# Attention and FFN kernel: the first pair's row maxima taken in two parts, and the query sums moved to the ends of odd halves

## The reference, cut to what matters

```python
def _attn_ref(q, k, v):              # q, k, v: 4 x 8 x 1152 x 64
    q_pool = q.reshape(B, H, S // 2, 2, D).mean(axis=3)
    scores = scale * np.matmul(q_pool, k.transpose(0, 1, 3, 2))
    scores = scores - np.max(scores, axis=-1, keepdims=True)
    attn = np.exp(scores)
    attn = attn / (np.sum(attn, axis=-1, keepdims=True) + 1e-09)
    return np.matmul(attn, v)
...
x = attn_out.transpose(0, 2, 1, 3).reshape(B * S, H * D)     # 2304 x 512
h = x @ w_in                                                  # 512 x 2048
g = np.where(h > 0.0, h, np.exp(np.minimum(h, 0.0)) - 1.0)
x = g @ w_out                                                 # 2048 x 512
logits = x @ phi                                              # 32 slots
```

## Time and profile before

| | |
|---|---|
| median of 3 executions | 971.53 us (969.62 to 973.15) |
| the profiled execution, its own time | 970.04 us |
| its span, from the first to the last instruction | 968.3 us |
| start to the first score (L528) | 25.49 us |
| attention | to about 475 us |
| PE, DVE, ACT, POOL busy, share of the span | 95%, 54%, 41%, 37% |

### The profile page before, as it was taken

The page is one execution under the profiler, slowest core; times in us unless marked ns, Lnnn a source line. Parts: engine busy times, 40 slices in busy tenths (PEclk is TensorE's granted clock), DMA queues, the critical chain, the costliest instruction groups (busy, mean ns, idle before and its releaser), DMA issues.

```text
span 968.3 us, 16639 instructions
## 1 busy us (share of the span) xinstructions
PE 918.9 (95%) x6450; PEld 704.1 (73%) x6450; DVE 520.5 (54%) x918; ACT 395.6 (41%) x733; POOL 362.3 (37%) x263
## 2 busy tenths in 40 slices
PE   3999999999999999999999999999999999999794
PEld 2556665656555666565799999999999999999332
DVE  6767666767676667665464443443433433434333
ACT  2655555555555555547442322322322322322102
POOL 1788878787887787888200000000000000000000
PEclk9999999999999999999999999999999999999998
DMA  6022022221211222302330000200000000457895
GB/s 231 25 75 71 30 73 74 75 72 52 75 59 41 74 75 74 91 1 70 105 111 1 1 1 1 88 1 1 1 1 1 1 1 1 144 218 257 310 376 196
DMA packets 36127, 76.32 MB, mean 79 GB/s; under 512 B 2897, under 2 KB 11217, under 8 KB 36049
## 3 DMA queue, kind: packets, MB, share of 16 engines
q1 hardware_dynamic: 36048, 75.26, 22.3%
HBM read 70.53 MB, written 4.72 MB: 78 GB/s over the span
## 4 chain that ended last, share of the span: by engine, by line
PE 49%; POOL 2%; DVE 1%; ACT 0%; DMA 0%; issue 0%; POOLq 0%; ACTq 0%; DVEq 0%
PE psum L611 7%; PE psum L593 7%; PE psum L595 7%; PE psum L612 7%; PE psum L613 7%; PE psum L594 7%; POOL acc L1258 2%; PE psum L688 2%; PE psum L723 1%; PE psum L644 1%; PE psum L650 1%; PE psum L626 0%; PE psum L544 0%; DMA out<-ob 0%; PE psum L631 0%
## 5 line engine op out<-in xcount | busy, mean ns | idle before, releaser
L1258 POOL TENSOR_TENSOR acc<-acc,pt 128x576 f32<-128x576 f32 x220 | 312.6, 1421 | 64.1 <-ACT pt L810 39.0
L810 ACT ACTIVATE pt<-psum 128x576 f32<-128x576 f32 x288 | 182.8, 651 | 135.3 <-PE psum L531 135.2
L530 PE MATMUL psum<-qs,kraw 64*128 64x288 f32 x576 | 182.8, 403 | 0.0
L531 PE MATMUL psum<-qs,kraw 64*128 64x288 f32 x576 | 182.7, 403 | 0.0
L984 DVE TENSOR_REDUCE mx<-psum 128x1 f32<-128x512 f32 x256 | 162.2, 677 | 18.0 <-PE psum L496 16.7
L544 PE MATMUL psum<-pt,vs 128*64 128x288 f32 x1152 | 153.6, 412 | 0.0
L1150 DVE TENSOR_SCALAR gf<-gf 128x384 f32<-128x384 f32 x96 | 34.6, 360 | 195.7 <-ACT gf L926 195.7
L611 PE MATMUL psum<-gh,W 128*128 128x384 f32 x384 | 133.4, 347 | 0.0
L926 ACT ACTIVATE gf<-psum 128x384 f32<-128x384 f32 x96 | 47.2, 492 | 200.8 <-PE psum L595 200.2
L612 PE MATMUL psum<-gl,W 128*128 128x384 f32 x384 | 128.5, 335 | 0.0
L595 PE MATMUL psum<-xh,W 128*128 128x384 f32 x384 | 128.5, 335 | 0.0
(11 more groups left out here) (128 smaller groups left out, 1324.3 us busy)
## 6 DMA issues: line engine op xcount, KB each, us to landing
ring<-in_w SPq DMA_DIRECT2D x32, 1024.0 KB, 7.4
qraw<-in_qT SPq DMA_DIRECT2D x16, 576.0 KB, 4.9
kraw<-in_kT SPq DMA_DIRECT2D x16, 576.0 KB, 3.7
vs<-in_v SPq DMA_DIRECT2D x16, 576.0 KB, 3.8
out<-ob SPq DMA_DIRECT2D x9, 512.0 KB, 6.2
wst<-in_w_in SPq DMA_DIRECT2D x16, 256.0 KB, 2.8
wst<-in_w_out SPq DMA_DIRECT2D x16, 256.0 KB, 3.1
sel<-in_selection SPq DMA_DIRECT2D x1, 96.0 KB, 6.8
```

Source lines behind the costliest of these rows:

```text
L530: mm(lo, kraw[0:64, p % NB, keys], qs[0:64, p % NB, q], start=False, stop=True).then_inc(s_Ta, 1)
L531: mm(hi, kraw[64:P, p % NB, keys], qs[64:P, p % NB, q], start=False, stop=True).then_inc(s_Tb, 1)
L810: act.activation(pt[:, i % NPT, :, :], t_pair(("T", h, kt))[:, :, 0:HALF], ACT.Exp, scale=SCALE)\
L1258: pool.tensor_tensor(a, first, pt[:, i % NPT, :, :], ALU.add).then_inc(s_acc, 1)
```

## The change

The FFN has chunks of 384 tokens before and after. What differs is the start of the attention and the place of the query sums.

Ahead of the first score stand only the units 0 to 5 and 8 of pair 0, which give the maxima of the first 384 queries of both heads. These are negated, transposed and copied by themselves (`first_negated_max`, `first_max_rows`, `read_first_rows`). Half 0 needs queries 0 to 287 only. The units 6, 7, 9 and 10 of pair 0 are worked off in the steps of half 0, and the rows of the other 192 queries follow at its end (`second_max_rows`, `read_second_rows`), ahead of half 1. The units of pair 1 move back accordingly. `queries(1)` now stands behind the first maxima, and ACT rounds these queries between the exps of half 0. From pair 3 on, `queries(p)` stands at the end of the odd half of pair p - 3, ahead of the `normalize` of the next half; before, it stood at the end of the even half of pair p - 2.

```diff
     def s_items(h, at):
 
         p = h // 2
-        if h % 2 == 0:
-            ahead, units = 1, {0: (1,), 2: (2,), 4: (3,), LATE: (9,), 7: (4,), END: (5,)}
-            if h == 0:
-                units[0], units[1] = (0,), (1,)
+        if h == 0:
+            units = {0: ((0, 6),), 2: ((0, 7),), 4: ((1, 0),), LATE: ((0, 9), (0, 10)), 6: ((1, 1),), 7: ((1, 2),),
+                     END: ((1, 3),)}
+        elif h == 1:
+            units = {0: ((1, 4),), 2: ((1, 5),), 3: ((1, 6),), 4: ((1, 7),), LATE: ((1, 9), (1, 10)), 6: ((1, 8),),
+                     7: ((2, 0),)}
...
+        def first_max_rows():
+            item = ("TRA", 0)
+            for freed in r_free[item]:
+                pe.wait_ge(*freed)
+            pe.wait_ge(s_nma, 1)
+            pe.wait_ge(d_eye, 16)
+            for j in range(3):
+                ins = nc.tensor.transpose(r_bank(item)[0:65, j * P:(j + 1) * P], nm2[:, 0, j, :], ident[:, :])
+            ins.then_inc(s_TRa, 1)
...
+                    pe.wait_ge(s_trca, 1)
+                else:
+                    pe.wait_ge(s_trc, 3 * p + 3)
                 pe.wait_ge(s_qs, p + 1)
                 pe.wait_ge(d_k[p % NB], 16 * (p // NB + 1))
+            if (h, kt) == (1, 0):
+                pe.wait_ge(s_trc, 3)
...
+        def read_first_rows():
+            act.wait_ge(s_TRa, 1)
+            act.wait_ge(s_zero, 3)
+            act.copy(nmT[0:65, 0, 0:3 * P], r_bank(("TRA", 0))[0:65, 0:3 * P]).then_inc(s_trca, 1)
...
-        queries_round(1)
-        last_queries_round(1)
-        read_rows_of_max(0)
+        read_first_rows()
...
+                if (h, kt) == (0, 1):
+                    queries_round(1)
+                if (h, kt) == (0, 3):
+                    last_queries_round(1)
...
+        def first_negated_max():
+            dve.wait_ge(s_red, red_at["S", 0, FIRST_UNITS[-1]] + 2)
+            dve.wait_ge(s_zero, 3)
+            dve.tensor_reduce(nm2[:, 0, 0:3, 0:65:64], mx[:, 0, 0:3, :, :], AX.X, ALU.max, negate=True).then_inc(s_nma, 1)
...
         queries(0)
-        for u in range(3):
+        for u in FIRST_UNITS:
             reduce_item(("S", 0, u))
+        first_negated_max()
         queries(1)
-        for u in range(3, NU):
-            reduce_item(("S", 0, u))
-        negated_max(0)
...
-            for item in s_items(h, END):
-                reduce_item(item)
-            if h % 2 == 0 and p + 2 < NP:
-                queries(p + 2)
+            reduce_items(s_items(h, END))
+            if h == 0:
+                queries(2)
+            if h % 2 and p + 3 < NP:
+                queries(p + 3)
```

More of the change, by code:

```diff
@@ L205, in rows_at @@
         return h % 2 and h // 2 + 1 < NP
-    r_items = [("S", 0, u) for u in range(NU)] + [("TR", 0)]
+    r_items = [("S", 0, u) for u in FIRST_UNITS] + [("TRA", 0)]
     t_items = []
@@ L217, in soft_moe_kernel @@
         r_items += s_items(h, END)
+        if h == 0:
+            r_items.append(("TRB", 0))
         if rows_at(h):
             r_items.append(("TR", h // 2 + 1))
+    last_unit = {item[1]: item for item in r_items if item[0] == "S"}
     t_at = {item: n for n, item in enumerate(t_items)}
     def banks_of(item):
-        return 1 if item[0] == "SUM" or item[0] == "S" and item[2] == NU - 1 else 2
-    FIRST = 2 * (NU - 1) + 1
+        return 1 if item[0] in ("SUM", "TRA", "TRB") or item[0] == "S" and item[2] == NU - 1 else 2
+    FIRST = 2 * len(FIRST_UNITS)
     FIRST_BANKS = (0, 1, 2, 3, 4, 5)
@@ L240, in soft_moe_kernel @@
                 freed_by[bank] = (s_sum, item[1] + 1)
-            elif item[0] == "TR":
+            elif item[0] == "TRA":
+                freed_by[bank] = (s_trca, 1)
+            elif item[0] in ("TR", "TRB"):
                 freed_by[bank] = (s_trc, 3 * item[1] + 3)
@@ L511, in max_rows, with second_max_rows @@
             nc.tensor.transpose(hi[0:65, 0:P], nm2[:, p % 2, 4, :], ident[:, :]).then_inc(s_TR, 1)
+        def first_max_rows():
[7 more added lines that the diff above has]
+            ins.then_inc(s_TRa, 1)
+        def second_max_rows():
+            item = ("TRB", 0)
+            for freed in r_free[item]:
+                pe.wait_ge(*freed)
+            pe.wait_ge(s_nm, 2)
+            for j in range(2):
+                ins = nc.tensor.transpose(r_bank(item)[0:65, j * P:(j + 1) * P], nm2[:, 0, 3 + j, :], ident[:, :])
+            ins.then_inc(s_TR, 1)
         def scores(h, kt):
@@ L546, in times_v @@
                 ins.then_inc(s_pv, 1)
-        for u in range(NU):
+        for u in FIRST_UNITS:
             ring_item(("S", 0, u))
-        max_rows(0)
+        first_max_rows()
         pe.wait_ge(s_one, 1)
@@ L787, in last_queries_round, with read_second_rows @@
             act.copy(bdq[64:P, b, 64:P], qs[64:P, p % NB, 4 * P:SQ]).then_inc(s_bdq, 1)
+        def read_first_rows():
+            act.wait_ge(s_TRa, 1)
+            act.wait_ge(s_zero, 3)
+            act.copy(nmT[0:65, 0, 0:3 * P], r_bank(("TRA", 0))[0:65, 0:3 * P]).then_inc(s_trca, 1)
+        def read_second_rows():
+            bank = r_bank(("TRB", 0))
+            act.wait_ge(s_TR, 1)
+            act.copy(nmT[0:65, 0, 3 * P:4 * P], bank[0:65, 0:P]).then_inc(s_trc, 1)
+            act.copy(nmT[0:1, 0, 4 * P:SQ], bank[0:1, P:P + 64]).then_inc(s_trc, 1)
+            act.copy(nmT[64:65, 0, 4 * P:SQ], bank[64:65, P + 64:2 * P]).then_inc(s_trc, 1)
         def read_rows_of_max(p):
```

33 lines of the change are left out of this document (20 added, 13 removed).

## The result

The changed kernel takes 959.18 us (median of four, 959.12 to 960.34), the kernel before beside it 970.94 (four, 969.62 to 973.15). The ratio is 0.9879 with a 95% interval of 0.9859 to 0.9900: 1.2% faster. The forecast was 959.3. The profiled executions lie closer together: 959.24 against 970.04, and in their spans 957.5 against 968.3, which is 10.8 us. That 959.18 agrees so closely with 959.3 is luck: the gain came out 1.4 us smaller than forecast, and the base that it was taken from lay 1.5 us above its profiled execution.

What follows compares the result with a forecast made beforehand. It took the chain before the first score and, in steady state, PE's stall behind even-half query sums as the bounds; 9.0 + 3.2 = 12.2 us off the 971.53 us median gave 959.3 us, range 955.8 to 963.9.

Steps and rivals of the forecast that it cites:

- Thirteen sums at 0.69 us: Steady part: even halves 2 to 26 each lose their query sum and gain 0.69 us, 9.0 us in all.
- The cover of 0.63 us: End of odd halves: the 1.36 us sum fits DVE's 1.99 us wait, leaving 0.63 us, so costs nothing.
- The lateness that would undo the gain: Rival, odd-half ends: a sum 0.94 us beyond the cover cancels the gain; 1.5 us gives 978.8 us; chance 0.03.
- The first score at 19.0 us: Start: with fewer reductions, transposes and copies ahead, the first score starts about 19.0 us, 6.5 earlier than 25.49.
- 3.2 us kept of 6.5: Start: of the 6.5 us, 3.2 remain at the first unit of half 2, at 47.1 or 47.2 instead of 50.38.
- DVE's work behind the first maxima: Start: DVE's work from 17.3 us up to the first product of half 2, forecast at 24.5 us without pauses.
- with these it comes to 46.8, and I add 0.3: Start: DVE's list ending at 41.8 plus 5.0 us of pauses, plus 0.3 for unit 8's bank wait, gives 47.1.
- I let the durations fall as long after the new start: Half 0: PE's matmuls shorten as long after the new start as before, at about 22 us; nothing added for ring waits.
- The Trainium skill's rule on clocks that drop between groups: Half 0: short idle times between matmul groups cycling PSUM banks slow the clock; sum 9 us, not 12.2; not followed.
- the rival: Start gives nothing: PE stays slow through half 0, or the ring stalls every unit of half 1; 962.5 us, chance 0.16.
- its 12.2 us: Whole kernel: total gain, 9.0 us from the moved sums plus 3.2 us from the start.

Runs made afterwards that it cites:

- the sums alone: Kernel before with only the query sums of pairs 3 to 15 moved to the ends of odd halves, old start kept: 961.71 us, ratio 0.9901.
- the run with the sum twice: Changed kernel with each query sum of pairs 3 to 15 taken twice in a row at the end of odd halves: 962.77 us, ratio 0.9916.
- the two traces with an early clock: Changed kernel with sums of pairs 3 to 15 back at even ends (967.29 us), and changed kernel rerun unedited (959.45 us); short matmul durations from about 20.5 us.
- the repeated run: The changed kernel measured once more with no edit: 959.45 us, ratio 0.9876.
- the kernel before with fillers: Kernel before plus idle matmuls of ones on PE around pair 0's eleven units and until the negated maxima: 971.50 us, ratio 0.9993.
- the changed kernel with 8 fillers: Changed kernel plus idle matmuls of ones on PE before and between the first seven units, 8 behind the last: 957.66 us, ratio 0.9859.
- with 18: Changed kernel plus the same idle matmuls, 18 instead of 8 behind unit 8, until the first negated maxima: 956.74 us, ratio 0.9852.

## Why the prediction was right, and where it was not

- *Thirteen sums at 0.69 us.* Right: 27.15 in the run of the sums alone. In the changed kernel the term is 8.5 and not 9.0, for the two exps that come late (0.56 us together). The prediction had no step for them. The mechanism is shown by PE's thirteen waits for DVE, which are there with the sums at even ends, with the old start and with the new, and gone in the changed kernel and in the sums alone.
- *The cover of 0.63 us.* Right: 0.78. The lateness that would undo the gain was under-sized, since the run with the sum twice lost only 0.24 us a pair with the product 0.55 late.
- *The first score at 19.0 us.* Right: 18.34, or 18.9 without the landing.
- *3.2 us kept of 6.5.* The mechanism was right, the size was not: 1.7 us in the profiled execution, 2.8 to 2.9 in the two traces with an early clock. DVE's work behind the first maxima was forecast at 24.5 us. Measured it is 31.72 from 16.56 to 48.28, less pauses of 0.46, 1.87, 1.10, 0.17, 2.86 and 0.49, so 24.8. The step that failed is the pauses: "with these it comes to 46.8, and I add 0.3" allowed 5.3 us, and they were 6.95. In the repeated run they were 5.75, so 1.2 of the missing 1.65 us is the clock, and the rest is the wait of 0.49 for the products at the end.
- *The clock.* "I let the durations fall as long after the new start" took as fixed what isn't: 20.1 to 20.6 us in three traces, 22.8 to 23.3 in three others, with the same program up to there. The Trainium skill's rule on clocks that drop between groups ("TensorE: Matmul & The Clock Gate", section "A second HAM failure mode: psum-queue depth-cycling") did not come true in the changed kernel: from 23.3 us on no score matmul took 0.68 again, with waits of up to 1.07 us between units. In the kernel before with fillers it did: behind PE's wait of 1.60 us for a bank the granted clock fell to 0.50 at 14.6 us. And in the changed kernel with 8 fillers it fell behind a pause of 2.01 us before the transposes, while with 18 the pause was 0.85 and the clock stayed. So the rival was a real one; the waits in half 0 of the changed kernel were shorter than these two.
- *The medians.* They give 11.8 to 12.2 us where the marks and spans give 10.8. The prediction took its 12.2 us off a median, 971.53, that lies 1.5 us above its profiled execution (970.04), and the gain fell 1.4 us short: 1.5 at the start and 0.5 at the sums, less 0.6 for the landing. So the two errors cancel. Of 31 executions of the kernel before in the later comparisons, the 24 with a mean granted clock of 0.989 or 0.990 took 971.2 to 973.1 us, the 7 with 0.992 or 0.994 took 969.6 to 970.7; the profiled one has 0.994. The clock is lost near the end. In every trace it falls once to 0.50 around 900 us, for a stretch of different length, before (its columns as above):

```profile
912.10:915.30 3.20, 3.20 (x20) 0.60 (x16) 0.86 (x4) 0.09 (x1) 0.00 (x0) 0.50 0.03 5
```

  in the changed kernel:

```profile
897.20:903.80 6.60, 4.45 (x26) 1.56 (x27) 4.34 (x13) 0.28 (x1) 0.00 (x0) 0.50 0.44 169
```

  and in the same run again:

```profile
894.50:904.50 10.00, 7.08 (x35) 1.94 (x37) 5.25 (x14) 0.87 (x2) 0.00 (x0) 0.50 0.49 189
```

  In the seven microseconds ahead of these stretches PE was busy for 3.3 us (before) and 4.4 us (changed). From mark 28 to the end the six traces with a stretch of 3.4 or 6.8 us take 549.0 to 549.2 us. Of the eight with 10.2 us four take 550.3, two 550.6 and 550.9 (both with one more stretch at 0.50 near 943 us), but one takes 549.1 and one 548.7. So a long stretch goes with a long tail in most traces and not in all, and no run shows it to be the cause.

## What to carry to other kernels

Look for a repetition of the loop that lacks the work in question, such as the last one: it prices a move better than any sum of durations, here to 0.01 us a period. Work on the engine that isn't the bound belongs into the place where that engine waits, but ask first what the work itself waits for: a query sum was free at the ends of odd halves, and cost more than it brought in half 0, where its load had not landed. When a start is shortened by putting work off, count what the ring of buffers makes of the backlog, and measure several executions before believing the first microseconds: one of them here came and went with the clock.

## What the runs showed of the hardware that I had not expected

- The time at which PE's matmuls go from 0.68 to 0.40 us varied by some 3 us between executions of the same program, and moved the mark in half 1 by 0.8 to 1.2 us. The granted clock says nothing of it: in these traces it reads 1.00 from 0 to 30 us, at the long durations too.
- Matmuls of no use before the first score, carried on until DVE's maxima were there, brought 1.6 us at the mark in half 1 against an early rise and 2.8 against a late one. The median fell by 2.7 us (959.45 to 956.74, whose ranges don't touch). With ten fewer of them PE paused for 2.01 us instead of 0.85, and the short durations were lost again.
- A wait of PE for the ring, 1.60 us, was followed by ten microseconds at a granted clock of 0.50 in the kernel before with fillers; waits of up to 1.07 us in the changed kernel were followed by none.
- Near 900 us the granted clock falls to 0.50 for 3.4, 6.8 or 10.2 us from one execution to the next, each time behind microseconds in which PE is half idle. The tail is 549.0 to 549.2 us with the two shorter ones and mostly, not always, 1.2 us or more longer with the longest.
- Two ACT instructions start 0.24 and 0.29 us late at fixed places of the program, in all ten traces with the new start and in none of the four without.
